# An attention and two MLPs on one core: the first eight heads' first queries as whole float32 products, the first MLP's operations at other places, and 40 unread products at the start

## The chip, the cores and the metric

The kernel runs on one core of a Trainium2 chip. The time is the device time of one execution in microseconds (us). Three executions of the kernel before took 917.24, 921.59 and 922.11 us; their median, 921.59 us, is what the changed kernel is compared with. Lower is better.

## The reference

Inputs are float32. Attention has 4 batches of 8 heads, 576 positions and a head size of 64; its output is the input of the first MLP, and that MLP's output the input of the second.

```python
cum = np.cumsum(np.maximum(s, 0.0), axis=-1)
scores = q @ k.T / 8 + np.minimum(-(cum[..., :, None] - cum[..., None, :]), 0.0)
attn = softmax(np.where(causal, -1e9, scores))       # over the keys
x = (attn @ v), transposed to 2304 tokens x 512
# first MLP: 512 -> 1024 -> 512
h = x @ w_in
solu = h * softmax(h)
x = (layernorm(solu) * g_ln) @ w_out
# second MLP: 512 -> 2048 -> 512
h = x @ w2_in
out = (h * np.clip(h + 3, 0, 6) / 6) @ w2_out
```

## The kernel before

ScalarE (ACT in the profile) writes the high part, and VectorE (DVE) or GpSimd (POOL) the low part. For queries and keys this is `split_qk` (ACT L1124, then POOL L610 and L613), for values `split_v` (POOL L627, L629), for the transposed probabilities `copy_probs` (ACT L1155) and `split_probs` (DVE L953), for the first MLP's weights `split_w_in` and `split_w_out`, and for its input `split_x` (DVE L1004 writes `xs_hi`, POOL L655 `xs_lo`).

**Units, items, slots.** A unit is a pair of heads with their first 256 queries (first kind) or the other 320 (second kind). A batch has four units of the first kind and then four of the second. A unit of the first kind has two items and one of the second five, 112 items in all. Each engine runs the same loop over slots n. In slot n TensorE transposes the probabilities of item n (`transpose_probs`, L736), multiplies them with the values of earlier units (`weighted_values`, L761) and computes the scores of item n+2 (L717, L720 and L722; L720 adds the causal mask). VectorE adds the decay bias and takes the row maximum of item n+1 (`row_max`, L944), and ScalarE takes the exponentials of item n+1 (`exp_row`, L1132). ScalarE and VectorE add up the two parts of the output (`copy_corr` L1163, `add_parts` L973), and a unit's output is scaled two slots after its last item (`scales_slot`). Each engine works strictly through its own list and waits on semaphores.

**The first MLP** is woven into the same loop: 18 steps t of 128 tokens, each cut in six pieces r = 0 to 5 on the slots that `STARTS` gives. Pieces 0 to 2 are `hidden` (L794, 24 products in a step). The row maximum (`max1`) comes in piece 3, the exponential (`exp1`, ACT L1182) and `solu` (DVE L1014 to L1022) in piece 4, and the squares (`square`, ACT L1188) in piece 5. The norm and the transposes (L807) follow in the next step, and pieces 3 to 5 hold the projection of an earlier pair of steps (`project`, L823). The second MLP follows as a loop of its own after the slots; all its products lie in L843 to L862.

A step's input can be split no earlier than the unit that completes its tokens is scaled:

```python
X_AT = {max(STARTS[t] - 3, whole_at(t)): t for t in range(NT)}
SPLIT_X_AT = {n + 1: t for n, t in X_AT.items()}
```

VectorE makes `xs_hi` in slot `X_AT`, and GpSimd makes `xs_lo` one slot later. `whole_at` is slot 10 for t = 0, slot 30 for t = 2, slot 58 for t = 6 and slot 114 for t = 15; `STARTS` of these four steps are 12, 31, 59 and 115. For the other steps the start lies four to eighteen slots behind `whole_at`.

**The start.** SyncE (SP) issues all loads. The bias of the first unit is spread over the partitions by two products (L869) after the cumulative sum (L923); all later ones are loaded from DRAM (`load_bias`).

Of the kernel before, what the change touches and what calls it, by code (L numbers as in the profile page):

```python
# [14 lines left out]
P = 128  # L15
# [63 lines left out]
A_WORDS = 4 * DH + 6 * ST + 6 * NQ * DH + 2 * BANK + SEQ + 3 * P + BANK + NQ * P + 2 * P_COLS  # L79
# [4 lines left out]
STARTS = [12, 21, 31, 37, 44, 51, 59, 65, 71, 77, 84, 90, 96, 102, 109, 115, 121, 127, 133]  # L84
# [10 lines left out]
W_IN_FROM, W_OUT_FROM, EARLY_FROM = 3, 24, 120  # L95

OWN = HEADS
# [18 lines left out]

def half_of(u):

    return u % 2 if FIRST_KIND[u] else 0

def units_of_half(u):

    return [m for m in range(u + 1) if half_of(m) == half_of(u)]

def load_of(u, e):
    return 2 * u + e
# [11 lines left out]
def buffer_of(load):  # L140

    return 3 + load if load < OWN else (load - OWN) % 3

def loads_of_buffer(load):

    return 1 if load < OWN else (load - OWN) // 3 + 1
# [10 lines left out]
for _u in range(UNITS):  # L158
    for _e in range(2):
        if load_of(_u, _e) < OWN:  # L160
            _n = max(-3, load_of(_u, _e) - 5)
        elif _u == PAIRS:
# [9 lines left out]
for _u in range(UNITS):  # L172
    for _e in range(2):
        VALUES_SLOT[_u, _e] = BASE[_u] + (1 + _e if not FIRST_KIND[_u] else _e)
        VALUES_AT.setdefault(VALUES_SLOT[_u, _e], []).append((_u, _e))
# [17 lines left out]
def build(nc, qk0, qk1, v_rows, s, w_in, w_out, g_ln, w2_in, w2_out, cum_dram, out):  # L193
    with ExitStack() as ctx:
# [27 lines left out]

# [17 lines left out]
        v_sp = [sb(a_region, f"v_sp{p}", [P, NQ, 2, DH], F32R) for p in range(2)]  # L241
        v_raw = [sb(a_region, f"v_raw{p}", [P, NQ, DH]) for p in range(2)]
        bias = [sb(a_region, f"bias{p}", [P, BANK]) for p in range(2)]
# [3 lines left out]
        p_hi = sb(a_region, "p_hi", [P, P_COLS], F32R)  # L247
        with ExitStack() as early:
            cum = sb(early, "cum", [NH, SEQ])
            s_pos = sb(early, "s_pos", [NH, SEQ])  # L250
        p_lo = sb(a_region, "p_lo", [P, P_COLS], F32R)
# [5 lines left out]
        with ExitStack() as own:  # L257
            for p in range(3, 3 + OWN):
                qk_buffer(own, p, QW[1] + KN[1])
# [10 lines left out]
        es = sb(first, "es", [P, F1])  # L270
        xs_hi = sb(first, "xs_hi", [P, NC, P], F32R)
# [95 lines left out]
        qk_loaded = [sem(f"qk_loaded{p}") for p in range(3 + OWN)]  # L367

        v_loaded = [[sem(f"v_loaded{p}{i}") for i in range(2)] for p in range(2)]
        bias_loaded = [[sem(f"bias_loaded{p}{i}") for i in range(2)] for p in range(2)]  # L370
        bias_tail_loaded = sem("bias_tail_loaded")
        w_in_loaded = [sem(f"w_in_loaded{p}") for p in range(W_IN_PARTS)]
        w_out_loaded = sem("w_out_loaded")
# [17 lines left out]
        pT_ready = sem("pT_ready")  # L391
        pT_hi_done = sem("pT_hi_done")
# [13 lines left out]
        bias_spread = sem("bias_spread")  # L406
        bias_copied = sem("bias_copied")
# [48 lines left out]
        def bias_loads(u):  # L456

            return len(units_of_half(u)) - (1 if half_of(u) == half_of(0) else 0)
# [7 lines left out]
        def _(sp):  # L466
            def load_qk(u, e):
                load = load_of(u, e)
                p, c = buffer_of(load), kind(u)
                if load >= OWN + 3:  # L470

                    u_, e_ = (load - 3) // 2, (load - 3) % 2
                    if FIRST_KIND[u_] or e_ == 1:
                        sp.wait_ge(scores_ready, BASE[u_] + (e_ if FIRST_KIND[u_] else 4) + 1)
                    else:
                        sp.wait_ge(tail_half_ready, sum(not k for k in FIRST_KIND[:u_ + 1]))
# [3 lines left out]
            def load_bias(u, e):  # L480
                before = user_before(u)
# [4 lines left out]
                sp.dma_start(bias[e][:, at:at + n], cum_dram[h:h + 1, 0:n].to_broadcast([P, n])).then_inc(bias_loaded[e][half_of(u)], 16)  # L486
# [9 lines left out]

            def load_v(u, e):
                before = user_before(u)
                if before >= 0:
# [15 lines left out]
            load_qk(0, 0)  # L515
            load_qk(0, 1)
            load_qk(1, 0)
            sp.wait_ge(cum_done, 1)
            sp.dma_start(cum_dram, cum[:, :]).then_inc(cum_stored, 16)
            load_qk(1, 1)  # L520
            sp.wait_ge(cum_stored, 16)
            for e in range(2):
                load_bias(1, e)
            load_qk(2, 0)
            for e in range(2):
                load_v(0, e)
            load_qk(2, 1)
            load_qk(3, 0)
            for e in range(2):
# [784 lines left out]
```

## Time and profile before

| | |
|---|---|
| three executions | 917.24, 921.59, 922.11 us |
| median | 921.59 us |
| profiled execution | 918.19 us, of which span 916.4 us |
| TensorE (PE) busy | 845.5 us, 92% of the span |
| VectorE busy | 441.9 us, 48% |
| ScalarE busy | 412.8 us, 45% |
| GpSimd busy | 296.5 us, 32% |
| mean granted clock of TensorE | 0.976 |

The span runs from the first to the last instruction, and 1.8 us of the execution lie around it. The slots with the attention and the first MLP fill about the first 508 us, and the second MLP the rest.
### The profile page before, as it was taken

The numbers are of one execution on the slowest core, as the hardware profiler recorded it, in microseconds if no ns is written. First come the engines' busy times: TensorE is split into PE (matmuls) and PEld (weight loads), VectorE is DVE, ScalarE is ACT, GpSimd is POOL, SyncE is SP. The second block draws the span as 40 slices with busy tenths as digits, with TensorE's granted clock in tenths as the row PEclk, the third lists the DMA queues.
The fourth block names the chain that finished last, engine by engine and source line by source line (L and its number), as shares of the span: only waits on it lengthen the run. The fifth ranks groups of instructions, "written<-read, shape, count | busy, mean of one in ns | idle before, by whom it ended". The sixth has DMA issues, their size and how long they took to land.

```text
span 916.4 us, 13790 instructions
## 1 busy us (share of the span) xinstructions
PE 845.5 (92%) x4916; PEld 750.7 (82%) x4916; DVE 441.9 (48%) x1061; ACT 412.8 (45%) x911; POOL 296.5 (32%) x391
## 2 busy tenths in 40 slices
PE   7778779989899998999898999999999999999997
PEld 5566668888688887888787999989898999999996
DVE  3747767776676767667455232232322232332222
ACT  6745766657566566555223243232322232322222
POOL 7764466455644465453165253000000000000000
PEclk9789879999999999999999999999999999999999
DMA  7536434334434344331402040000000000000000
GB/s 232 176 111 208 119 97 141 96 99 125 124 95 115 91 115 123 108 113 40 137 2 92 1 138 1 35 1 1 35 0 1 35 1 1 35 1 1 35 1 34
DMA packets 39426, 66.84 MB, mean 73 GB/s; under 512 B 4480, under 2 KB 16512, under 8 KB 39360
## 3 DMA queue, kind: packets, MB, share of 16 engines
q1 hardware_dynamic: 39360, 65.97, 23.7%
q8 instruction: 40, 0.66, 0.3%
q14 instruction: 26, 0.21, 0.1%
HBM read 61.16 MB, written 4.79 MB: 72 GB/s over the span
## 4 chain that ended last, share of the span: by engine, by line
PE 69%; DVE 10%; ACT 9%; issue 5%; POOL 4%; DMA 2%; SPq 0%; DVEq 0%; ACTq 0%; POOLq 0%
PE psum L794 9%; PE psum L843 7%; PE psum L845 7%; PE psum L861 7%; PE psum L844 7%; PE psum L862 7%; PE psum L860 7%; PE psum L761 4%; PE psum L823 3%; PE psum L736 3%; ACT prob L1132 3%; ACT p_hi L1155 2%; DVE es L1018 2%; PE psum L807 2%; PE psum L722 2%
## 5 line engine op out<-in xcount | busy, mean ns | idle before, releaser
L1086 DVE SCALAR_TENSOR_TENSOR act<-act,psum 128x384 f32<-128x384 f32 x96 | 53.2, 554 | 286.8 <-ACT act L1240 286.8
L1240 ACT ACTIVATE act<-psum,three 128x384 f32<-128x384 f32 x96 | 55.9, 582 | 285.7 <-PE psum L845 285.7
L843 PE MATMUL psum<-x_hi,w_hi 128*128 128x384 f32 x384 | 129.5, 337 | 0.9 <-DVE x_lo L1044 0.9
L845 PE MATMUL psum<-x_hi,w_lo 128*128 128x384 f32 x384 | 129.5, 337 | 0.0
L844 PE MATMUL psum<-x_lo,w_hi 128*128 128x384 f32 x384 | 129.0, 336 | 0.0
L862 PE MATMUL psum<-w_hi,g_lo 128*128 128x512 f32 x288 | 113.9, 395 | 0.0
L861 PE MATMUL psum<-w_lo,g_hi 128*128 128x512 f32 x288 | 113.7, 395 | 0.0
L860 PE MATMUL psum<-w_hi,g_hi 128*128 128x512 f32 x288 | 112.0, 389 | 0.0
L953 DVE TENSOR_TENSOR p_lo<-psum,p_hi 128x512 fp32r<-128x512 f32 (+2 forms) x128 | 71.9, 572 | 79.5 <-ACT p_hi L1155 79.0
L1155 ACT ACTIVATE p_hi<-psum 128x512 fp32r<-128x512 f32 (+2 forms) x128 | 62.3, 500 | 96.0 <-PE psum L736 63.1
L610 POOL TENSOR_TENSOR qk_hi<-qk_raw,qk_hi 64x256 fp32r<-64x256 f32 (+1 forms) x64 | 57.0, 891 | 125.3 <-ACT qk_hi L1124 124.1
L823 PE MATMUL psum<-lnT_hi,w_out_hi 128*128 128x256 f32 x288 | 83.2, 289 | 9.9 <-DVE xT L1040 9.7
L1132 ACT ACTIVATE prob<-prob,nmax 128x128 f32<-128x128 f32 (+4 forms) x144 | 83.2, 580 | 12.2 <-DVE nmax L944 12.0
L736 PE MATMUL psum<-ident,prob 128*128 128x128 f32 x400 | 67.9, 290 | 20.7 <-ACT prob L1132 17.6
L823 PE MATMUL psum<-lnT_lo,w_out_hi 128*128 128x256 f32 x288 | 82.2, 285 | 0.0
L823 PE MATMUL psum<-lnT_hi,w_out_lo 128*128 128x256 f32 x288 | 82.2, 285 | 0.0
L736 PEld LDWEIGHTS psum<-ident,prob 128*128 128x128 f32 x400 | 49.3, 147 | 33.2 <-ACT prob L1132 28.4
L843 PEld LDWEIGHTS psum<-x_hi,w_hi 128*128 128x128 f32 x384 | 72.1, 188 | 5.3 <-DVE x_lo L1044 1.1
L844 PEld LDWEIGHTS psum<-x_lo,w_hi 128*128 128x128 f32 x384 | 72.1, 188 | 4.0
L722 PE MATMUL psum<-qk_lo,qk_hi 128*128 128x128 f32 (+2 forms) x192 | 73.8, 388 | 0.0
L794 PE MATMUL psum<-w_in_hi,xs_hi 128*128 128x512 f32 x144 | 60.9, 423 | 12.7 <-POOL xs_lo L655 12.7
L613 POOL TENSOR_TENSOR qk_lo<-qk_raw,qk_hi 128x256 fp32r<-128x256 f32 (+1 forms) x64 | 70.9, 1108 | 5.0
(95 smaller groups left out, 1881.6 us busy)
## 6 DMA issues: line engine op xcount, KB each, us to landing
qk_raw<-qk SPq DMA_DIRECT2D x32, 480.0 KB, 3.5
qk_raw<-qk SPq DMA_DIRECT2D x32, 256.0 KB, 2.7
bias<-cum_dram SPq DMA_DIRECT2D x32, 256.0 KB, 3.9
v_raw<-v_rows SPq DMA_DIRECT2D x32, 160.0 KB, 3.1
bias_tail<-cum_dram SPq DMA_DIRECT2D x32, 144.0 KB, 3.8
out<-out_sb SPq DMA_DIRECT2D x6, 768.0 KB, 3.5
w_raw<-w_in SPq DMA_DIRECT2D x16, 256.0 KB, 3.2
w_raw<-w_out SPq DMA_DIRECT2D x16, 256.0 KB, 4.1
```

The source lines that it names most:

```text
L722: last = pe.matmul(ps, q, qk_lo[p][:, keys], start=False, stop=(part != 0))
L736: last = pe.transpose(dst, prob[:, src:src + P], ident[:, :])
L794: last = pe.matmul(bank(h_bank(t) + half), x, w, start=(n % 12 == 0), stop=(n % 12 == 11))
L823: last = pe.matmul(bank(L_BANK, PJW), w, x, start=(n == 0), stop=(n == 23))
L843: pe.matmul(ps, w2_hi[f][:, cols], xh, start=(c_ == 0), stop=False)
L844: pe.matmul(ps, w2_hi[f][:, cols], xl, start=False, stop=False)
L845: last = pe.matmul(ps, w2_lo[f][:, cols], xh, start=False, stop=(c_ == NC - 1))
L860: pe.matmul(bank(4 + k), gh, w2_hi[f][:, NC * P:], start=(f == 0), stop=False)
L861: pe.matmul(bank(4 + k), gh, w2_lo[f][:, NC * P:], start=False, stop=False)
L862: last = pe.matmul(bank(4 + k), gl, w2_hi[f][:, NC * P:], start=False, stop=(f == NF2 - 1))
L1132: sc.activation(p, p, ACT.Exp, scale=-1.0, bias=nmax[:, u % 2, col:col + 1], accum_out=rsum[:, u % 2, col:col + 1]).then_inc(exp_done, 1)
L1155: sc.activation(hi, ps, ACT.Copy).then_inc(pT_hi_done, 1)
```

## The change

Three things are changed together.

**Plain units.** The first four units (`PLAIN = 4`; batch 0, all eight heads, first 256 queries) are no longer split. Their queries and keys are loaded as float32 with the two heads of a pair on top of each other (`qk_plain`, 128 partitions) in place of each head twice. TensorE multiplies whole float32 operands with 64 rows, and the bias comes in as a further product of `cum_parts` (high and low part of the cumulative sum) with a column of `heads`. The probabilities are copied once, by VectorE (`copy_plain`), and multiplied as float32 with the loaded values (`v_pair`). The output is copied once, by ScalarE (`copy_sums`), and `add_parts` falls away. The two products L869 and their copies go, the full cumulative sum is made after the first `copy_plain` (`sum_all`), and the loads come in another order.

**First MLP.** `STARTS` changes. In the slots `exp1` and `square` come behind the copy of the probabilities and the exponentials; `max1` and `solu` come right behind `row_max`, and `solu` in piece 5 in place of 4. `square` writes to SBUF (`squares`), and `hidden` waits for `solu` in place of `square`. `w_out` is loaded in eight parts of 256 KB in place of one of 2048 KB and split in slots 27 to 34 (24 to 31 before); `w_in` is split in slots 6 to 13 (3 to 10 before).

**Head of the program.** TensorE begins with 40 products of 128 columns whose result nobody reads.

```diff
-STARTS = [12, 21, 31, 37, 44, 51, 59, 65, 71, 77, 84, 90, 96, 102, 109, 115, 121, 127, 133]
+STARTS = [13, 25, 33, 39, 45, 54, 60, 66, 72, 78, 84, 90, 96, 103, 110, 116, 122, 129, 135]
-W_IN_FROM, W_OUT_FROM, EARLY_FROM = 3, 24, 120
+W_IN_LOAD = 2
+W_IN_FROM = 6
+W_OUT_LOAD = 15
+W_OUT_FROM = 27
+PLAIN = 4
...
+                    if u < PLAIN:
+                        rows = slice(0, P) if e is None else slice(e * DH, (e + 1) * DH)
+                        q = qk_plain[u][rows, q_at:q_at + P]
+                        for lo_, hi_ in [(0, w)] if w <= BANK else [(0, w // 2), (w // 2, w)]:
+                            pe.matmul(psum[:, at + lo_:at + hi_], q, qk_plain[u][rows, QW[c] + lo_:QW[c] + hi_],
+                                      start=True, stop=False)
+                            if n <= 1:
+                                pe.wait_ge(cum_parts_done, n + 1)
+                            h = head_of(u, e)
+                            last = pe.matmul(psum[:, at + lo_:at + hi_], heads[rows, h:h + 1].broadcast_to([DH, P]),
+                                             cum_parts[rows, lo_:hi_], start=False, stop=hi_ <= diag0)
...
+                    if u < PLAIN:
+                        p, v_at = plain_values(u)
+                        last = pe.matmul(psum[:, o_at + q:o_at + width], v_pair[p][:, v_at + j, :, :].rearrange("p a d -> p (a d)"),
+                                         p_plain[:, src:src + width - q], start=(j == 0), stop=(j == blocks - 1))
...
-                    wait(pe, sq_done, t - 1 if t >= NT - 2 else t)
+                    wait(pe, solu_done, t - 1 if t >= NT - 2 else t)
...
-            pe.wait_ge(cum_done, 1)
-            for e in range(2):
-                pe.matmul(bank(H_BANK + e, CUT), ident[0:NH, e:e + 1].broadcast_to([NH, P]), cum[:, 0:CUT],
-                          start=True, stop=True).then_inc(bias_spread, 1)
+            for _ in range(40):
+                pe.matmul(bank(H_BANK + 1, P), ident_bf[:, :], mask_bf[:, :], start=True, stop=True)
...
+                if r == 3:
+                    max1(t)
+                if r == 5:
+                    solu(t)
...
-                if 0 <= n < ITEMS:
+                if 0 <= n < PLAIN_ITEMS:
+                    copy_plain(n)
+                    if n == 0:
+                        sum_all()
+                elif 0 <= n < ITEMS:
                     split_probs(n)
...
-                if r == 3:
-                    max1(t)
-                if r == 4:
-                    solu(t)
```

TensorE's list at its start, before (L869 spreads the bias; `qk_hi3` and `qk_lo3` are parts of one head's queries and keys):

```order
L869 MATMUL psum<-cum,ident 128x256 x2
L717 MATMUL psum<-qk_hi3 128x128
L720 MATMUL psum<-mask_bf,ident_bf 128x128
L722 MATMUL psum<-qk_lo3,qk_hi3 128x128
L717 MATMUL psum<-qk_hi3 128x256
L720 MATMUL psum<-mask_bf,ident_bf 128x128
L722 MATMUL psum<-qk_lo3,qk_hi3 128x256
```

The same place in the changed kernel (L974 are the unread products, L796 the float32 ones, L801 the bias):

```order
L974 MATMUL psum<-mask_bf,ident_bf 128x128 x40
L796 MATMUL psum<-qk_plain0 128x128
L801 MATMUL psum<-cum_parts,heads 128x128
L805 MATMUL psum<-mask_bf,ident_bf 128x128
L796 MATMUL psum<-qk_plain0 128x256
L801 MATMUL psum<-cum_parts,heads 128x256
L805 MATMUL psum<-mask_bf,ident_bf 128x128
```

For each tile one float32 product and one bias product stand where two float32r products stood.

ScalarE's list around the first step's exponential, before (L1182 is `exp1`, L1155 and L1132 the attention's copy and exponential):

```order
L1132 ACTIVATE prob,rsum<-prob,nmax 128x384
L1182 ACTIVATE es,esum1<-psum,nmax1 128x1024
L1155 ACTIVATE p_hi<-psum 128x3x128
L1132 ACTIVATE prob,rsum<-prob,nmax 128x512
L1163 ACTIVATE xT<-psum 64x320
L1124 ACTIVATE qk_hi0<-qk_raw0 128x960
L1188 ACTIVATE psum,sq_sum<-es,neg_mu 128x1024
L1155 ACTIVATE p_hi<-psum 128x4x128
```

The same operations in the changed kernel, at the third step (L1328 is `exp1`, L1296 and L1273 the attention's):

```order
L1296 ACTIVATE p_hi<-psum 128x384
L1273 ACTIVATE prob,rsum<-prob,nmax 128x128
L1273 ACTIVATE prob,rsum<-prob,nmax 128x256
L1328 ACTIVATE es,esum1<-psum,nmax1 128x1024
L1265 ACTIVATE qk_hi1<-qk_raw1 128x512
L1322 ACTIVATE w_out_hi<-w_out_raw,g_sb 128x512
L1296 ACTIVATE p_hi<-psum 128x384
```

The exponential of the MLP stood ahead of the slot's attention work and now stands behind it.

VectorE's list at the first step's `solu`, before (L1014 to L1022 are `solu`, L953 is the low part of the probabilities, L944 the row maximum):

```order
L944 ISA prob,nmax<-psum,bias0 128x512
L944 ISA nmax 128x1
L953 TENSOR_TENSOR p_lo<-psum,p_hi 128x3x128
L973 TENSOR_TENSOR xT<-psum,xT 64x320
L959 TENSOR_SCALAR den<-rsum 128x5
L963 RECIPROCAL rden<-den 128x5
L1014 TENSOR_SCALAR den1<-esum1 128x1
L1016 RECIPROCAL rden1<-den1 128x1
L1018 SCALAR_TENSOR_TENSOR es,solu_sum<-psum,rden1,es 128x1024
L1022 TENSOR_SCALAR neg_mu<-solu_sum 128x1
```

The same place in the changed kernel (L1150 to L1158 are `solu`, L1089 the low part, L1062 the row maximum):

```order
L1062 ISA prob,nmax<-psum,bias00 128x512
L1062 ISA nmax 128x1
L1150 TENSOR_SCALAR den1<-esum1 128x1
L1152 RECIPROCAL rden1<-den1 128x1
L1154 SCALAR_TENSOR_TENSOR es,solu_sum<-psum,rden1,es 128x1024
L1158 TENSOR_SCALAR neg_mu<-solu_sum 128x1
L1089 TENSOR_TENSOR p_lo<-psum,p_hi 128x3x128
L1109 TENSOR_TENSOR xT<-psum,xT 64x320
```

`solu` stood behind the low part of the probabilities and now stands ahead of it.

## Rows read from the trace of the kernel before

**Rows 1.** The page, busy time of each engine.
```profile
PE 845.5 (92%) x4916; PEld 750.7 (82%) x4916; DVE 441.9 (48%) x1061; ACT 412.8 (45%) x911; POOL 296.5 (32%) x391
```

**Rows 2.** Stretches: bounds, length, busy time by engine, PEclk, DMA share, GB/s.
```profile
11.00:22.10 11.10, 9.69 (x44) 8.15 (x43) 5.32 (x21) 9.34 (x28) 8.98 (x18) 1.00 0.90 292
...
49.40:56.20 6.80, 5.02 (x13) 3.67 (x14) 0.00 (x0) 0.00 (x0) 2.95 (x3) 0.50 0.03 8
...
104.00:110.90 6.90, 4.62 (x21) 4.21 (x20) 5.35 (x18) 4.69 (x14) 4.05 (x6) 0.51 0.43 125
...
117.70:127.90 10.20, 6.27 (x21) 5.16 (x22) 7.31 (x19) 5.42 (x15) 8.32 (x14) 0.50 0.20 53
...
233.70:237.10 3.40, 3.40 (x11) 2.60 (x10) 0.18 (x1) 0.00 (x0) 2.19 (x4) 0.50 0.00 0
...
452.20:455.60 3.40, 3.40 (x12) 2.71 (x10) 0.00 (x0) 0.00 (x0) 0.00 (x0) 0.50 1.00 350
...
508.00:910.00 402.00, 402.00 (x2044) 364.79 (x2043) 111.33 (x215) 116.15 (x227) 23.97 (x10) 1.00 0.05 18
```

**Rows 3.** Waits, whole span: total us, times, longest.
```profile
PE psum L736 <- ACT prob L1132: 17.6, 23, 2.3
PE psum L794 <- POOL xs_lo L655: 12.7, 4, 3.8
...
ACT psum L1188 <- DVE neg_mu L1022: 37.0, 17, 3.1
...
ACT es L1182 <- DVE nmax L1009: 26.5, 15, 2.8
```

**Rows 4.** Timeline of TensorE: start, length, instruction; transposes of slots 0, 2, 3, 8.
```profile
9.90 0.90 PE L736 MATMUL psum<-ident,prob 128*128 128x128 f32 x3 [0.30 <-ACT prob L1132]
...
15.34 0.90 PE L736 MATMUL psum<-ident,prob 128*128 128x128 f32 x3 [0.22 <-ACT prob L1132]
...
17.70 0.90 PE L736 MATMUL psum<-ident,prob 128*128 128x128 f32 x3 [0.22 <-ACT prob L1132]
...
34.19 0.84 PE L736 MATMUL psum<-ident,prob 128*128 128x128 f32 x3
```

**Rows 5.** Timeline of ScalarE in slot 2.
```profile
16.28 0.49 ACT L1155 ACTIVATE p_hi<-psum 128x384 fp32r<-128x384 f32 x1 [0.47 <-PE psum L736]
...
17.55 0.62 ACT L1124 ACTIVATE qk_hi<-qk_raw 128x512 fp32r<-128x512 f32 x1
```

**Rows 6.** Timeline of TensorE: float32 products, scores of head 0, values.
```profile
4.80 2.04 PE L869 MATMUL psum<-cum,ident 32*128 32x256 f32 x4 [4.80 <-DVE cum L923]
6.77 0.47 PE L717 MATMUL psum<-qk_hi 128*128 128x128 f32 x1
...
8.16 0.31 PE L717 MATMUL psum<-qk_hi 128*128 128x128 f32 x1
...
18.25 0.56 PE L761 MATMUL psum<-p_hi,v_sp 128*128 128x256 f32 x1
...
19.14 0.52 PE L761 MATMUL psum<-p_hi,v_sp 128*128 128x256 f32 x1
```

**Rows 7.** Timeline of TensorE: the four waits for `xs_lo`.
```profile
51.18 0.80 PE L794 MATMUL psum<-w_in_hi,xs_hi 128*128 128x512 f32 x1 [3.77 <-POOL xs_lo L655]
...
124.15 0.79 PE L794 MATMUL psum<-w_in_hi,xs_hi 128*128 128x512 f32 x1 [2.95 <-POOL xs_lo L655]
...
233.38 0.51 PE L794 MATMUL psum<-w_in_hi,xs_hi 128*128 128x512 f32 x1 [3.56 <-POOL xs_lo L655]
...
451.64 0.50 PE L794 MATMUL psum<-w_in_hi,xs_hi 128*128 128x512 f32 x1 [2.42 <-POOL xs_lo L655]
```

**Rows 8.** Timeline of GpSimd ahead of the first of these waits' end.
```profile
48.51 1.40 POOL L613 TENSOR_TENSOR qk_lo<-qk_raw,qk_hi 128x576 fp32r<-128x576 f32 x1
49.87 1.26 POOL L655 TENSOR_TENSOR xs_lo<-xT,xs_hi 128x512 fp32r<-128x512 f32 x1
```

**Rows 9.** Chain that ended last: one `hidden` piece of eight products.
```profile
455.78 1.86 PE psum L794 x8
```

**Rows 10.** Timeline of VectorE: the long instruction of `solu`.
```profile
446.59 1.28 DVE L1018 SCALAR_TENSOR_TENSOR es<-psum,rden,es 128x1024 f32<-128x1024 f32 x1
```

More of the change, by code:

```diff
@@ L140, in buffer_of, with los, seconds, plain_values @@
 def buffer_of(load):
-    return 3 + load if load < OWN else (load - OWN) % 3
+    return load % 3
 def loads_of_buffer(load):
-    return 1 if load < OWN else (load - OWN) // 3 + 1
+    return load // 3 + 1
+def los(n):
+    return LOS_BEFORE[n] - LOS_BEFORE[PLAIN_ITEMS]
+def seconds(u):
+    return sum(not k for k in FIRST_KIND[PLAIN:u + 1])
+def plain_values(u):
+    if FIRST_KIND[u]:
+        return u // 2 % 2, u % 2 * 2
+    return u % 2, 0
 SUMS_AT = {}
@@ L157 @@
 SPLIT_AT = {}
-for _u in range(UNITS):
+for _u in range(PLAIN, UNITS):
     for _e in range(2):
-        if load_of(_u, _e) < OWN:
-            _n = max(-3, load_of(_u, _e) - 5)
-        elif _u == PAIRS:
+        if _u == PLAIN:
             _n = BASE[_u] - 5 + _e
@@ L190, with build @@
 SPLIT_X_AT = {n + 1: t for n, t in X_AT.items()}
-def build(nc, qk0, qk1, v_rows, s, w_in, w_out, g_ln, w2_in, w2_out, cum_dram, out):
+def build(nc, qk0, qk1, plain0, plain1, v_rows, v_pairs, s, w_in, w_out, g_ln, w2_in, w2_out, cum_dram, out):
     with ExitStack() as ctx:
@@ L257, in build @@
         with ExitStack() as own:
-            for p in range(3, 3 + OWN):
-                qk_buffer(own, p, QW[1] + KN[1])
+            qk_plain = [sb(own, f"qk_plain{u}", [P, QW[kind(u)] + KN[kind(u)]]) for u in range(PLAIN)]
         w_out_hi = sb(first, "w_out_hi", [P, NF1, DM], F32R)
@@ L456, in bias_loads @@
         def bias_loads(u):
-            return len(units_of_half(u)) - (1 if half_of(u) == half_of(0) else 0)
+            return sum(bias_place(m) == bias_place(u) for m in range(PLAIN, u + 1))
         def tokens(u):
@@ L475, in load_qk @@
                     else:
-                        sp.wait_ge(tail_half_ready, sum(not k for k in FIRST_KIND[:u_ + 1]))
+                        sp.wait_ge(tail_half_ready, seconds(u_))
                 w = QW[c] + KN[c]
@@ L549, in _ @@
                             load_bias_tail(u)
-                for u in range(2, UNITS):
+                for u in range(PLAIN, UNITS):
                     for e in range(2):
@@ L1211, in _ @@
                 t, r = STEP_AT.get(n, (None, None))
[L1212 to L1216 removed]
+                if PLAIN_ITEMS <= n < ITEMS:
                     copy_probs(n)
@@ L1221, in _ @@
                 for u, e in SUMS_AT.get(n, ()):
-                    copy_corr(u, e)
+                    if u < PLAIN:
+                        copy_sums(u, e)
+                    else:
+                        copy_corr(u, e)
+                if r == 4:
+                    exp1(t)
+                if r == 5:
+                    square(t)
                 if r in (1, 2) and t >= 1:
                     copy_ln(t - 1, r - 1)
+                for u, e in SPLIT_AT.get(n, ()):
+                    split_qk(u, e)
                 if W_OUT_FROM <= n < W_OUT_FROM + NF1:
@@ L1289, with pairs @@
     values = np.concatenate([v, np.zeros((NH, NQ * P - SEQ, DH), np.float32)], axis=1)
+    values = values.reshape(NH, NQ, P, DH).transpose(0, 2, 1, 3)
+    def pairs(x):
+        return x[:HEADS].reshape(PAIRS, 2 * DH, x.shape[2])
+    first = np.concatenate([qT[:, :, :CUT], kT[:, :, :CUT]], axis=2)
+    second = np.concatenate([qT[:, :, CUT:cut], tails, kT], axis=2)
     def twice(x):
@@ L1295 @@
     arrays = {
-        "qk0": twice(np.concatenate([qT[:, :, :CUT], kT[:, :, :CUT]], axis=2)),
-        "qk1": twice(np.concatenate([qT[:, :, CUT:cut], tails, kT], axis=2)),
-        "v_rows": values.reshape(NH, NQ, P, DH).transpose(0, 2, 1, 3),
+        "qk0": twice(first),
+        "qk1": twice(second),
+        "plain0": pairs(first),
+        "plain1": pairs(second),
+        "v_rows": values,
+        "v_pairs": values[:HEADS].reshape(PAIRS, 2, P, NQ, DH).transpose(0, 2, 3, 1, 4),
         "s": s.reshape(NH, SEQ),
```

259 lines of the change are left out of this document (166 added, 93 removed).

## The prediction

> **What bounds the kernel now.** The page comes first: TensorE is busy 92% of the span and no other engine reaches half [rows 1]. A table of stretches then shows that this share is made of two parts. From 508 to 910 us TensorE is busy 402.00 of 402 us at full clock [rows 2]; that is the second MLP, which the change leaves as it is. What can be won lies in the slots, the first 508 us. There TensorE loses time in two ways, and both have rows. It waits: 17.6 us for exponentials of the attention and 12.7 us for `xs_lo` of the first MLP [rows 3]. And it runs at half clock, 1.2 GHz: six named stretches [rows 2]. In 11.0 to 22.1 us products run at the half-clock spacing (a slot's scores and transposes repeat every 2.36 us, 15.34 to 17.70 [rows 4]); the table's 1.00 there only means that no change had been recorded. The other five stretches of half clock come behind idle time: 49.4 to 56.2 behind a wait of 3.77 us, 233.7 and 452.2 inside or just behind waits of 3.56 and 2.42 us [rows 2, 7].
>
> The timeline of the first slots shows a closed loop: ScalarE copies the transposed probabilities 0.47 us after the transposes are done, then takes two exponentials, 1.27 us from 16.28 to 17.55 [rows 5], and TensorE's next transposes wait for these. Nine slots' starts, slot 0 at 9.90 and slot 8 at 34.19, are 24.3 us apart [rows 4].
>
> **Term 1, slots 0 to 8.** The copy of the probabilities leaves ScalarE, so its exponentials no longer wait for the transposes, and the loop is cut. ScalarE also loses eight splits of queries and keys of 0.62 us [rows 5], GpSimd all its work for these heads, and SyncE loads half the bytes of queries and keys in a stretch whose transfers fill 0.90 of the DMA engines [rows 2]. What binds then is TensorE itself. Two float32 products of 256 columns started at 4.80, and the next product could start at 6.77 [rows 6], so one costs up to 0.98 us at half clock; I take 0.95, and 0.48 for 128 columns. A head's scores then cost 0.48 + 0.95 for the products, about 0.55 for two bias products and 0.18 for two masks (both from the 1.39 us that six products took, 6.77 to 8.16 [rows 6]), 2.2 us in place of 1.39. A head's values cost 0.95 + 0.48 = 1.4 us in place of 0.89 (18.25 to 19.14 [rows 6]). With transposes (0.55) and scales a slot holds 4.2 us of TensorE at half clock and 2.1 us at full clock, 1.3 and 0.65 us more than before. These are the two bounds: 8 x 2.1 + 1.5 us of starting latency = 18.3 us, a gain of 6.0; or 8 x 4.2 + 1.5 = 35.1 us, a loss of 10.8. Which of them comes is the clock's affair. The 40 products need no data, can start when the constants are there, and end about when the first scores can start; behind them TensorE's list is dense for the first time in this program. Before, it was busy 9.69 of 11.1 us in short products and rose to full clock only at 22.1. I take the full clock, -6.
>
> The Trainium skill (FP8 and Floating Point Precision, TensorE Precision Notes) says that true float32 takes four passes through the array. By it 256 columns would be 4 x 256 / 1.2 GHz = 0.85 us, and the eight slots at half clock an estimated 2 us cheaper than by the row. The row agrees within what stands between the two products.
>
> **Term 2, slots 8 to 13.** Before, slot 8 began at 34.19 and the first `hidden` piece at 51.18, behind a wait of 3.77 us [rows 4, 7]; GpSimd was late, with queries' low part and `xs_lo` back to back until 51.1 [rows 8]. It enters this stretch with no backlog now, and the step starts in slot 13, three behind `whole_at` 10, not two. The wait goes, 3.8 us, and its eight products run at full clock, another 1.8 us (they took 1.86 us elsewhere [rows 9]). The splits of `w_in` that now lie here add to ScalarE what they took three slots earlier before; I take 0.6 back. -5.
>
> **Term 3, the other waits for `xs_lo`.** They stand at t = 2, 6 and 15, 2.95 + 3.56 + 2.42 = 8.9 us [rows 7]. These are exactly the steps that started one slot behind `whole_at`, the slot in which GpSimd only makes `xs_lo`. The new starts lie 3, 2 and 2 slots behind. Between nothing (the wait moves along, if all that TensorE has in the added slot is done early) and all 8.9, I take -7, since a slot holds a piece of TensorE work of 1.9 us [rows 9] besides the attention.
>
> **Term 4, half clock behind them.** In the stretches from 104.0, 117.7, 233.7 and 452.2 TensorE is busy 4.62 + 6.27 + 3.40 + 3.40 = 17.7 us at half clock [rows 2]; all at full clock would give 8.8. With fewer and shorter waits I take -5; the lower bound is nothing.
>
> **Term 5, ScalarE's list.** `square` and `exp1` hold ScalarE back 37.0 and 26.5 us in waits [rows 3], with the attention's copy and exponentials behind them. Put behind these they cost the attention nothing. But only 17.6 us of TensorE's time hang on exponentials, a part of them in the first slots. -3, between 0 and -10. The load of `w_out` in parts shortens no wait that I find on the chain: 0. Unread products end before the first scores: 0.
>
> **Term 6, work moved later.** Steps 0 to 2 ended in slot 36 and now end in slot 38. Two pieces of 1.9 us leave a stretch where TensorE waits in any case and are done where it is full: +4.
>
> **Sum.** -6 - 5 - 7 - 5 - 3 + 4 = -22. The profiled execution took 918.2 us, and gives 896. It lies 3.4 us below the median, from which the sum gives 900. I say 898.
>
> **Rivals.**
> *The first slots stay at half clock.* For it: 9.69 us busy of 11.1 did not raise the clock before. Against: float32 products stream four times the columns. Term 1 turns from -6 to +11: 915. Chance 0.12.
> *The waits move along and ScalarE binds.* Slots 8 to 36 are full of exponentials, splits and copies, so TensorE, with less to do there, waits for them at half clock; terms 3 to 5 give -5 rather than -15: 908. Chance 0.12.
> *The other side, slower.* `solu` (1.28 us [rows 10] and three short instructions, some 1.8 us) now stands ahead of the low part of the probabilities, for which the next transposes wait; so are late the exponentials' consumers behind them. Fifteen steps share slots with attention: up to 27 us. Where all of it reaches TensorE the sum is +5, 925. It decides from about 1.5 us a step. Against: ScalarE's copy, which the low part needs too, covers about 0.9 us, and TensorE has a 1.9 us projection piece in that slot. Chance 0.08.
> *More comes back.* All waits of terms 3 to 5 and all half clock: -37, 883. Chance 0.08.
>
> **Numbers.** The likeliest case has 0.60, and its own range is 889 to 907. The range 882 to 916 holds it and the first two rivals and leaves out the slower one. Half a per cent, 4.6 us, is what a measurement here can tell from no change. Faster than 917 are the likeliest case, most of the first two rivals and the last: 0.87. Within 0.5% the edge of the first rivals: 0.06. Slower 0.07.
>
> **What would show it.** Slot 8's transposes near 28 us, not near 43; products at full spacing from about 8 us on. ScalarE's waits before `square` and `exp1` nearly gone. No wait for `xs_lo` of over 1 us, and no fall of the clock at the starts of steps 2, 6 and 15. The last slot ending some 20 us before 508, and then 402 us as before. Wrong would make me: half clock until 20 us; VectorE late with the low part in the slots of piece 5, seen as a wait of the transposes for it; or new waits of TensorE for exponentials in slots 13 to 36.

## The result, and the profile after

The changed kernel takes 882.36 us (median of 4 runs: 881.93, 882.01, 882.71 and 890.40), the kernel before 921.84 us beside it. The ratio is 0.9604, with a 95% interval of 0.9541 to 0.9666: 39 us faster, where the prediction said 898 and a range of 882 to 916. The profiled execution took 882.01 us, with a span of 880.2; its counterpart before took 918.19, so the two traces differ by 36 us.

The page of the changed kernel, busy time of each engine; beside it stands [rows 1]:

```profile
PE 839.7 (95%) x4968; PEld 748.3 (85%) x4968; DVE 435.9 (50%) x1059; ACT 405.9 (46%) x893; POOL 282.0 (32%) x361
```

TensorE is busy 6 us less in a span that is 36 us shorter: what went is idle time, and busy time at half clock. Its stretches (bounds, length, busy time by engine, PEclk, DMA share, GB/s); beside them [rows 2]:

```profile
7.00:28.20 21.20, 20.91 (x123) 15.57 (x123) 12.73 (x53) 12.99 (x42) 5.96 (x7) 1.00 0.65 220
40.70:47.50 6.80, 6.07 (x20) 5.47 (x21) 2.50 (x8) 3.73 (x9) 4.99 (x5) 0.50 0.35 109
95.30:102.10 6.80, 6.32 (x30) 5.50 (x29) 6.25 (x20) 5.48 (x16) 4.46 (x8) 0.50 0.32 83
105.50:115.70 10.20, 7.10 (x27) 6.08 (x28) 6.87 (x21) 7.71 (x20) 7.83 (x12) 0.50 0.35 113
457.10:460.50 3.40, 3.37 (x11) 3.37 (x12) 1.06 (x2) 0.00 (x0) 0.00 (x0) 0.50 0.13 49
470.00:872.00 402.00, 402.00 (x2048) 364.99 (x2048) 111.46 (x216) 116.23 (x227) 24.02 (x10) 1.00 0.05 18
```

Full clock comes at 6.5 us instead of 22.1. The stretches of half clock at 233.7 and 452.2 are gone. One at the first step (40.7) and two in slots 29 to 33 (95.3 and 105.5) remain. The one at the start of the second MLP (457.1) is new; before, the clock stood at full there. The window of 402 us in the second MLP is again busy 402.00 of 402. The whole of it is longer than that window. Its first product came at 494.89 before, not at 508, and comes at 457.13 now:

```profile
494.89 0.45 PE L843 MATMUL psum<-x_hi,w_hi 128*128 128x384 f32 x1 [0.93 <-DVE x_lo L1044]
457.13 0.69 PE L949 MATMUL psum<-x_hi,w_hi 128*128 128x384 f32 x1 [2.60 <-DVE x_lo L1180]
```

So the slots are 37.8 us shorter, and what follows them is 1.6 us longer. Waits over the whole span (total us, times, longest), to be set beside [rows 3]:

```profile
ACT squares L1334 <- DVE neg_mu L1158: 14.6, 7, 4.3
PE psum L834 <- ACT prob L1273: 8.9, 13, 1.7
ACT es L1328 <- DVE nmax L1145: 7.9, 3, 2.9
PE psum L834 <- DVE p_lo L1089: 7.5, 6, 3.4
PE psum L929 <- DVE xT L1176: 5.3, 11, 0.6
PE psum L949 <- DVE x_lo L1180: 2.6, 1, 2.6
PE psum L900 <- POOL xs_lo L723: 0.8, 1, 0.8
```

The wait for `xs_lo` falls from 12.7 to 0.8 us, that for exponentials from 17.6 to 8.9. The low part of the probabilities is a wait that grew, from 2.5 us to 7.5. Three more rows of the kernel before, for the readings below:

```profile
PE psum L717 <- DVE nmax L944: 5.5, 5, 2.3
...
PE psum L773 <- DVE xT L973: 4.1, 6, 1.3
PE psum L736 <- DVE p_lo L953: 2.5, 3, 1.1
```

The first is TensorE's scores waiting for `row_max`, the second its products behind `add_parts`.

The timeline of TensorE at slots 0 and 8 (as [rows 4]) and at the starts of steps 0, 2, 6 and 15 (as [rows 7]):

```profile
10.12 0.55 PE L834 MATMUL psum<-ident,prob 128*128 128x128 f32 x3
...
28.25 0.49 PE L834 MATMUL psum<-ident,prob 128*128 128x128 f32 x3
...
44.41 0.77 PE L900 MATMUL psum<-w_in_hi,xs_hi 128*128 128x512 f32 x1
...
113.56 0.73 PE L900 MATMUL psum<-w_in_hi,xs_hi 128*128 128x512 f32 x1
...
212.39 0.48 PE L900 MATMUL psum<-w_in_hi,xs_hi 128*128 128x512 f32 x1
...
413.48 0.40 PE L900 MATMUL psum<-w_in_hi,xs_hi 128*128 128x512 f32 x1
```

No bracket stands behind the four products: none waits. Set against the trace before, slot 8 is 5.9 us early, step 0 6.8, step 2 10.6, step 6 21.0, step 15 38.2. So 17 us of the gain lie between steps 6 and 15 (212 to 413 us), where no head is plain and where the sum had only the wait of step 15 (2.42 us), the half clock behind the start of step 6 (1.7) and a part of term 5's 3 us.

### The profile page after: what moved, and what is told of

The parts are those of the page before. It is cut to its first block, busy times and chain, and to the rows that moved or that the text cites. A ratio compares the mean times of both kernels' runs of the same rounds, so it can differ in the third digit from the quotient of the medians.

```text
span 880.2 us, 13819 instructions
## 1 busy us (share of the span) xinstructions
PE 839.7 (95%) x4968; PEld 748.3 (85%) x4968; DVE 435.9 (50%) x1059; ACT 405.9 (46%) x893; POOL 282.0 (32%) x361
## 4 chain that ended last, share of the span: by engine, by line
PE 81%; ACT 7%; DVE 5%; issue 3%; POOL 3%; DMA 1%; ACTq 0%; DVEq 0%; POOLq 0%
PE psum L929 9%; PE psum L900 9%; PE psum L949 8%; PE psum L951 8%; PE psum L950 8%; PE psum L967 8%; PE psum L968 8%; PE psum L966 7%; PE psum L867 5%; PE psum L834 4%; PE psum L818 2%; PE psum L813 2%; ACT prob L1273 2%; PE psum L913 2%; ACT p_hi L1296 1%
## 5 line engine op out<-in xcount | busy, mean ns | idle before, releaser
L1296 ACT ACTIVATE p_hi<-psum 128x384 fp32r<-128x384 f32 (+1 forms) x120 | 58.7, 503 | 100.9 <-PE psum L834 66.5
L1273 ACT ACTIVATE prob<-prob,nmax 128x128 f32<-128x128 f32 (+4 forms) x144 | 83.4, 580 | 22.8 <-DVE nmax L1062 22.2
L1089 DVE TENSOR_TENSOR p_lo<-psum,p_hi 128x384 fp32r<-128x384 f32 (+1 forms) x120 | 67.1, 571 | 53.7 <-ACT p_hi L1296 53.7
L679 POOL TENSOR_TENSOR qk_hi<-qk_raw,qk_hi 64x384 fp32r<-64x384 f32 (+1 forms) x56 | 50.5, 901 | 103.3 <-ACT qk_hi L1265 101.7
L834 PE MATMUL psum<-ident,prob 128*128 128x128 f32 x400 | 64.8, 280 | 16.5 <-ACT prob L1273 8.9
L951 PEld LDWEIGHTS psum<-x_hi,w_lo 128*128 128x128 f32 x384 | 72.4, 189 | 0.0
L834 PEld LDWEIGHTS psum<-ident,prob 128*128 128x128 f32 x400 | 47.5, 143 | 26.7 <-ACT prob L1273 17.5
L682 POOL TENSOR_TENSOR qk_lo<-qk_raw,qk_hi 128x576 fp32r<-128x576 f32 (+1 forms) x56 | 67.7, 1208 | 4.4
L818 PE MATMUL psum<-qk_lo,qk_hi 128*128 128x288 f32 (+4 forms) x176 | 65.1, 375 | 0.0
```

Source lines behind the costliest of these rows:

```text
L682: pool.tensor_tensor(qk_lo[p][:, k_cols], qk_raw[p][:, k_cols], qk_hi[p][:, k_cols].bitcast(F32), ALU.subtract).then_inc(k_lo_done, 1)
L818: last = pe.matmul(ps, q, qk_lo[p][:, keys], start=False, stop=(part != 0))
L834: last = pe.transpose(dst, prob[:, src:src + P], ident[:, :])
L951: last = pe.matmul(ps, w2_lo[f][:, cols], xh, start=False, stop=(c_ == NC - 1))
L1273: sc.activation(p, p, ACT.Exp, scale=-1.0, bias=nmax[:, u % 2, col:col + 1], accum_out=rsum[:, u % 2, col:col + 1]).then_inc(exp_done, 1)
```

## The experiments

Each run was timed in up to five rounds beside the kernel before (medians of 919.3 to 921.8). The table has them all; the ratio is to the kernel before. The changed kernel has 0.9604 [0.9541, 0.9666]; its interval is wide because of its one run at 890.40, so differences of 5 us to it rest on the medians and on its other three runs.

| kernel | us | ratio, 95% interval |
|---|---|---|
| before + lists | 906.9 | 0.9845 [0.9823, 0.9868] |
| before + starts | 908.8 | 0.9864 [0.9844, 0.9884] |
| before + lists + starts | 888.0 | 0.9654 [0.9630, 0.9678] |
| the same + unread products | 890.1 | 0.9670 [0.9647, 0.9692] |
| changed, no unread products | 887.7 | 0.9656 [0.9630, 0.9681] |
| changed, old starts | 906.8 | 0.9865 [0.9835, 0.9895] |
| changed, old lists | 901.1 | 0.9806 [0.9766, 0.9846] |
| changed, ScalarE's list old | 910.2 | 0.9880 [0.9845, 0.9915] |
| changed, VectorE's list old | 902.8 | 0.9785 [0.9762, 0.9808] |
| changed, `solu` behind the low part | 891.7 | 0.9717 [0.9679, 0.9755] |
| changed, `split_x2` first | 886.0 | 0.9623 [0.9602, 0.9645] |
| the same, 24 more unread | 878.6 | 0.9540 [0.9520, 0.9560] |

**The new lists and starts alone.** The kernel before with the new lists and starts (its transposes' wait is written for the bank that each uses, since the first step now begins at an odd slot). It lacks the plain heads and the unread products, and also the smaller parts of the change: `square` into SBUF, `w_out` in eight parts, the later `w_in`. None of these smaller parts was timed alone.

```
-STARTS = [12, 21, 31, 37, ...
+STARTS = [13, 25, 33, 39, ...
 ScalarE:  -exp1, square ahead of copy_probs     +behind copy_corr
 VectorE:  -max1 (r 3), solu (r 4) behind invert +max1 (r 3), solu (r 5) ahead of split_probs
```

> The kernel before with two parts of the change alone: the new list of starts of the first MLP's steps, and the new places of `exp1`, `square`, `max1` and `solu` in the lists of ScalarE and VectorE. The first eight heads stay split, `square` still writes to PSUM, no unread products. By the terms of the prediction (3, 4, 5 and 6: -7 - 5 - 3 + 4) it gains 11 us on the kernel before, so 911, and the first heads hold the other 28 of the 39 us measured. The rival says that the order of the lists was priced too low: the two changed traces differ by 12 us more in slots 60 to 112 than the terms allow, where no plain head is; then this kernel gains 22 to 27 us, 895 to 900, and the first heads hold only the 11 us of terms 1 and 2.

It took 888.0, so it gains 31 us, three times the -11 of the terms and more than the rival's 22 to 27. Its waits:

```profile
PE psum L736 <- ACT prob L1132: 11.4, 19, 1.1
PE psum L736 <- DVE p_lo L953: 7.3, 6, 3.1
...
PE psum L823 <- DVE xT L1040: 3.1, 6, 0.6
...
PE psum L794 <- ACT psum L1188: 1.2, 1, 1.2
...
PE psum L794 <- POOL xs_lo L655: 0.8, 1, 0.8
```

They are nearly those of the changed kernel. The wait of `hidden` for `square` (L1188) is one that the changed kernel lacks, since its `hidden` waits for `solu`. Its first slots are those of before (slot 8 at 34.3), and the 6 us that it lacks to the changed kernel come from there: slot 12 stands 7.8 us behind the changed kernel's, slot 108 4.9, and the wait of 1.2 for `square` comes at 419.8.

**Each of the two alone.**

> The kernel before with the new places of `exp1`, `square`, `max1` and `solu` alone; old starts, split heads, `square` into PSUM, no unread products. Lists and new starts together gave 31 us. If each holds its own part, as the prediction's sum has it, this kernel and the one with the new starts alone add up to 31: by term 5 this one gives 3 us, 916; by the cost of taking the lists back out of the changed kernel (19 us, 6 of them in the first slots' clock) it gives 13: 906. The rival: they only pay together, since with steps one slot behind `whole_at` the waits for `xs_lo` stay whatever the lists; then it gives under 8 us, 912 to 919.

> The kernel before with the new list of starts alone (its transposes' wait is written for the bank that each uses, as in the changed kernel, since the first step now begins at an odd slot). By terms 3, 4 and 6: -7 - 5 + 4, 8 us, 911. By what was missing after the lists (31 less 13): 18 us, 901. No wait for `xs_lo` of over 1 us at steps 1, 2, 6 and 15 in either. The rival that they only pay together: 912 to 919.

The lists alone gain 14 us, the starts alone 12, and together 31: each has most of its worth alone, and 5 us come only with both. The waits of the kernel with the lists alone:

```profile
PE psum L794 <- POOL xs_lo L655: 12.6, 5, 3.5
PE psum L736 <- ACT prob L1132: 9.3, 14, 1.5
PE psum L736 <- DVE p_lo L953: 7.9, 7, 2.7
...
PE psum L823 <- DVE xT L1040: 3.3, 6, 0.6
```

The wait for `xs_lo` is untouched (12.7 before). Those for exponentials fall from 17.6 [rows 3] by 8.3 us. And waits fall that the prediction left out: that of the scores for `row_max` from 5.5 to 0.8, that behind `add_parts` (4.1) to nothing, and that of projections for `copy_x2` by 6.4 us, from this row of the kernel before:

```profile
PE psum L823 <- DVE xT L1040: 9.7, 12, 1.5
```

Against them the wait for the low part rises from 2.5 to 7.9.

The waits of the kernel with the starts alone:

```profile
PE psum L736 <- ACT prob L1132: 23.0, 25, 2.5
PE psum L823 <- DVE xT L1040: 9.2, 13, 1.4
...
PE psum L794 <- POOL xs_lo L655: 2.3, 2, 1.2
```

Here 10 us of waits for `xs_lo` went and 5 us of waits for exponentials came. This is the rival "the waits move along and ScalarE binds", and it is real as long as ScalarE has the old list. One of the two waits for `xs_lo` that stay is step 15's, 1.23 us at 441.57, where the expectation allowed no more than 1.

**The same two, taken out of the changed kernel.**

> The changed kernel with the old lists: `exp1` and `square` stand ahead of the attention's copy and exponentials on ScalarE, `max1` and `solu` behind the attention's work on VectorE, `solu` in piece 4 again. Plain heads, new starts and the unread products stay. Term 5 of the prediction prices the lists at 3 us: 885 to 886. The rival (lists priced too low) says 10 to 15 us: 892 to 898, with the waits of `square` back near 37 us and those of `exp1` near 26 us, and the loss spread over all steps rather than at their starts.

> The changed kernel with the old list of starts, but 13 for the first step (old: 12). Terms 3, 4 and 6 say that waits for `xs_lo` of up to 3.5 us come back at steps 2 and 6 and one of 2.4 at step 15, with half clock behind them, less the 4 us of work moved later: 8 us slower than the changed kernel, 890. The rival: the waits came from a slow GpSimd and ScalarE in the split heads and the old lists, which this kernel does not have; then xs_lo is in time even one slot behind, and the time is 880 to 884.

The old lists cost 19 us (901.1); the waits of `square` are 36.6 us again, those of `exp1` 26.2. The profiled execution took 905.1, 23 us more than the changed kernel's; in it the clock fell in the first slots (below), which is worth about 5 of the 23. The rest is spread as the rival had it: slots 60 to 108 take 192.8 us in place of 178.4. These slots in the changed kernel:

```profile
211.90:390.30 178.40, 175.50 (x1239) 157.20 (x1238) 132.87 (x346) 118.15 (x273) 101.41 (x139) 1.00 0.39 113
```

The same slots of the kernel with the old lists:

```profile
223.20:416.00 192.80, 178.95 (x1238) 158.69 (x1239) 132.99 (x349) 118.41 (x273) 99.28 (x138) 0.99 0.34 105
```

And TensorE's waits in it:

```profile
PE psum L929 <- DVE xT L1176: 9.1, 8, 1.8
PE psum L879 <- DVE xT L1109: 2.9, 3, 1.3
PE psum L834 <- ACT prob L1273: 1.0, 3, 0.4
```

TensorE's busy time differs by 3.5 us, its idle time by 11. And only 1.0 us of its idle time is a wait for exponentials. 12 of 13.9 us are waits for VectorE, for `copy_x2` and for the sums. VectorE itself stands in `split_probs` for `p_hi`, which ScalarE makes behind `exp1`. Its wait in these slots, with the old lists and then in the changed kernel:

```profile
DVE p_lo L1089 <- ACT p_hi L1296: 36.5, 36, 2.3
DVE p_lo L1089 <- ACT p_hi L1296: 23.3, 26, 2.5
```

That this wait is what makes `copy_x2` late is read from the order of VectorE's list, in which `copy_x2` of piece 4 comes right behind the low part.

The old starts cost 24 us (906.8), but 5.7 of it is a wait of the experiment's own: step 2 begins two slots earlier, and its first projection waits for `w_out_lo`, whose place was not moved. Waits for `xs_lo` are back at 9.4 us, and 23.9 us in a row run at half clock from 95.9. In its profiled execution, too, the clock fell in the first slots. Both theories priced it too low.

**One list at a time.** In the changed kernel one engine's list is put back, the other stays.

> The changed kernel with ScalarE's list alone put back: `exp1` and `square` ahead of the attention's copy and exponentials; VectorE's list stays new. If the loss of the old lists came through ScalarE (a wait at the head of its list delays the copy of the probabilities, so VectorE's low part, so the copies of x2 behind it, so the projections), most of the 18 us come back here: `max1` is early now, so `exp1` hardly waits, but `square` waits some 2 us a step for `solu`, which the same slot makes: 892 to 898. The rival: VectorE's own order is what matters, and this kernel takes 882 to 886.

> The changed kernel with VectorE's list alone put back: `max1` behind the attention's work in piece 3, `solu` behind it in piece 4; ScalarE's list stays new. The piece-5 slots then have no `solu` ahead of the low part. If that place cost something (the prediction's slower rival), this kernel is faster than the changed one by up to the waits for `p_lo`, 7.5 us: 875 to 882. If `solu` in piece 4 waits for an `exp1` that now stands at the end of ScalarE's list, VectorE stands some 2 us a step before the next slot's maximum, and it takes 887 to 898.

Both are worse than expected. With ScalarE's list alone put back the kernel takes 910.2, more than with both (901.1); with VectorE's alone 902.8, which is not to be told from both by the intervals, and where the slowest expectation ended at 898. Waits with ScalarE's list put back:

```profile
ACT squares L1334 <- DVE neg_mu L1158: 56.8, 18, 4.3
ACT es L1328 <- DVE nmax L1145: 7.9, 3, 2.9
...
PE psum L834 <- ACT prob L1273: 23.0, 21, 4.0
PE psum L929 <- DVE xT L1176: 5.3, 11, 0.6
```

`square` at the head of ScalarE's slot waits in every step for a `solu` of the same slot, 3.2 us on average (37.0 before in 17 waits), and the attention's copy and exponentials wait with it. The waits for `copy_x2`, though, are the changed kernel's 5.3 us: `max1` is early here, so `exp1` at the head of its slot hardly waits (7.9). It takes both halves of the old lists, `max1` late and `exp1` early, to delay `copy_x2`. With VectorE's list put back another wait grows, that of ScalarE's exponentials for the row maximum, 22.2 us in the changed kernel:

```profile
ACT prob L1273 <- DVE nmax L1062: 48.5, 45, 5.9
```

The two lists are one edit: `solu` may come early only where `square` comes late.

**Where `solu` stands on VectorE.**

```
                 if r == 3:
                     max1(t)
-                if r == 5:
-                    solu(t)
 ...
                 elif 0 <= n < ITEMS:
                     split_probs(n)
+                if r == 5:
+                    solu(t)
```

> The changed kernel with one line moved on VectorE: `solu` still in piece 5, but directly behind the low part of the probabilities instead of ahead of it. The prediction's slower rival said that `solu` ahead of the low part costs TensorE time. In the changed kernel's trace it does so at one place by 3.4 us (slot 31, piece 5 of step 1: the low part ends at 106.77 though its high part is there since 103.4), and the clock falls behind it; all waits for the low part come to 7.5 us. If these go and nothing takes their place: 876 to 879. The rival: `square` now waits longer for `solu` at the end of ScalarE's list, and the next slot's copy of the probabilities with it, as in the two kernels with one list put back; then 882 or above, up to 890.

It took 891.7, 9 us slower; four of six runs lie within 891.4 to 891.7. The other two took 900.6 and 900.7, and the trace is one of these, with 20.5 us of half clock in the first slots. In the changed kernel `solu` does hold up the low part in slot 31. TensorE's and VectorE's timeline there:

```profile
104.82 1.28 DVE L1154 SCALAR_TENSOR_TENSOR es<-psum,rden,es 128x1024 f32<-128x1024 f32 x1
...
106.22 0.55 DVE L1089 TENSOR_TENSOR p_lo<-psum,p_hi 128x384 fp32r<-128x384 f32 x1
...
106.92 0.88 PE L834 MATMUL psum<-ident,prob 128*128 128x128 f32 x3 [3.35 <-DVE p_lo L1089]
```

With `solu` behind, this slot takes 4.4 us instead of 6.0 (100.9 to 106.9). But the next takes 6.4 instead of 4.4, with a wait of 2.13 us for exponentials at its end: `square` comes later on ScalarE, then two splits, then `p_hi`. The wait moved and did not go. Over the whole kernel `square` waits 33.6 us (18 times) instead of 14.6 (7 times).

**The first slots and the clock.**

> The changed kernel without the 40 unread products at the head of TensorE's program, nothing else. If they are what brings the full clock to the first slots, the granted clock stays at 1.2 GHz beyond 6.5 us as long as the first slots' products do not raise it, and slot 8's transposes come later than 28.3: up to 43 us if it lasts through eight slots. If the plain products alone raise it, it rises 3 to 4 us after the first of them at about 7 us, and the loss is at most 1.5 us: 882 to 884, not to be told from the changed kernel by its time, but by slot 8's transposes at 29 to 30.

> The kernel before with the new lists and new starts (888.0) and the 40 unread products ahead of TensorE's first wait; the eight heads stay split. This asks whether the first heads' gain is the clock's alone. In this kernel's parent eight slots took 24.4 us, 34.3 at slot 8, and slots 4 to 8 were no faster than 0 to 4 though most of them ran at full clock. If ScalarE's loop sets the pace whatever the clock, slot 8 comes 2.3 us later, since the 40 products end at about 7.1 and the products that spread the bias start at 4.8 now: 36 to 37, and the time is 889 to 891. If the clock sets the pace, slot 8 comes at 31 to 32, and the time is 884 to 886, and the plain heads have little part in the gain.

The changed kernel without the unread products takes 887.7, with slot 8 at 37.0. Its first scores run at half clock though they start at 4.13, and the clock rises only at 31.0: from a product of 256 columns to the next instruction it is 0.34 us at 7.62 in the changed kernel, and 0.65 here. The split heads with unread products take 890.1, with slot 8 at 34.0, as without them (34.3). But the products didn't hold the clock there:

```profile
10.00:33.90 23.90, 22.02 (x94) 18.70 (x95) 14.89 (x52) 19.39 (x57) 20.34 (x34) 0.50 0.83 258
```

The same heads in the kernel without these products had full clock in a part of slots 4 to 8:

```profile
23.00:29.80 6.80, 4.20 (x30) 3.18 (x29) 5.44 (x16) 5.53 (x17) 6.40 (x9) 1.00 0.80 255
```

These four slots took 12.8 us in both. So where split heads had full clock they were no faster, and ScalarE's loop paced them there; eight split slots at full clock were seen in no trace. On top of the new lists and starts (0.9654) the rest of the change without unread products gives nothing (0.9656), nor do unread products alone (0.9670). All together gives 5.6 us in the medians (0.9604), which the intervals don't separate from nothing; three of four runs of the changed kernel lie at 881.9 to 882.7, and all of the three others at 886.8 or above.

**The head's clock is not settled by the 40 products.** Seven profiled executions ran kernels with the same first slots (the expectation below says six, and four falls; the count is seven and five). In two, the changed kernel's among them, the clock held from 7 us to about 40. In five it fell again between 10.3 and 11.6. The stretches of the kernel with `split_x2` first:

```profile
7.00:10.00 3.00, 3.00 (x19) 2.17 (x17) 0.64 (x4) 0.68 (x3) 0.00 (x0) 1.00 0.63 238
10.40:24.10 13.70, 13.70 (x47) 9.83 (x47) 6.12 (x24) 4.38 (x18) 0.40 (x1) 0.50 0.72 208
```

and of the same kernel with 24 more unread products:

```profile
7.00:10.00 3.00, 3.00 (x27) 2.33 (x25) 0.64 (x4) 0.99 (x4) 0.00 (x0) 1.00 0.68 257
10.40:24.10 13.70, 13.70 (x92) 10.55 (x90) 8.88 (x37) 8.79 (x29) 3.82 (x5) 1.00 0.69 193
```

The first of these kernels answers another question as well: the wait of 2.6 us for `x_lo` at the start of the second MLP.

```
+                if t == NT - 1 and r in (1, 2, 4, 5):
+                    split_x2(0, (1, 2, 4, 5).index(r))
                 if r == 4:
                     exp1(t)
                 if r == 5:
                     square(t)
```

(the same two lines ahead of `max1` on VectorE, and gone from their old places)

> The changed kernel with the split of the first transposed tokens for the second MLP (`split_x2`, four parts, in the last step alone) ahead of `exp1` and `square` on ScalarE and ahead of `max1` and `solu` on VectorE, instead of behind them. In the changed kernel its last part stands behind a wait of 3.20 us of `square` for `solu`; TensorE waits 2.60 us for it at 457.13 and then runs at half clock for 3.4 us. If that is the whole of it: the wait goes and the clock stays, 2.6 + 1.7 = 4.3 us, 878. The rival: the waits of the projection for the copies of x2 in the same step take its place, or the clock falls a little later: 881 to 883.

The wait and the half clock behind it are gone: from step 17's first product to the second MLP's first it takes 13.2 us instead of 16.0, and no fall of the clock stands there. But the median is 886.0, where 878 was expected. The first slots lost 6.2 us to the clock in the profiled execution, and the runs scatter, 882.3 to 887.3; the profiled one is the fastest of them. The last kernel adds, in TensorE's list:

```
                         scores(n + 2)
+                    if n < 0:
+                        for _ in range(12):
+                            pe.matmul(bank(H_BANK + 1, P), ident_bf[:, :], mask_bf[:, :], start=True, stop=True)
```

> The kernel with `split_x2` first, and 24 more unread products in TensorE's list: 12 behind the scores of slot 0 and 12 behind those of slot 1, 0.055 us each at full clock, 1.3 us in all. In six profiled executions of kernels with the same first slots the clock, up since about 7 us, fell again between 10.3 and 11.6 in four and held in two (the changed kernel's among them); where it fell slot 8 began at 34.4 or later in place of 28.3, and the end came some 5 us later. If the fall follows from too little work in the first scores, the added products hold the clock: slot 8 at 29.6 and 878 to 880 in nearly all runs. If it does not depend on them, the runs scatter as those of the kernel with `split_x2` first alone did, 882 to 887, plus up to 1.3: 883 to 889, and slot 8 stands at 29.6 or at 35.7 by the run.

All five runs lie between 877.6 and 879.8. In the profiled one slot 8 stands at 29.1, the clock holds until 40.0, and the 0.8 us that the products cost there have shrunk to 0.1 by slot 32. It beats the changed kernel by 4 us and the kernel before by 43. That the added work is what holds the clock follows from that one trace and from the narrow spread, beside a kernel that differs in nothing else and has no run below 882.3; which property of the products counts was not tried.

## Why the prediction was right, and where its terms were off

The direction, the mechanisms and the bound (TensorE's waits and half clock in the slots) were right. The sum of -22 was 14 us short of the profiled difference of 36. The rival "more comes back" gave 883 at a chance of 0.08, and that is what was measured, at the lower edge of the range. But the number was met in part by luck: that rival has all half clock gone, and some 24 us of it stayed in the slots (40.7, 95.3 and 105.5), while waits that no term names came on top.

**Terms 1 and 2, -6 and -5, measured -5.6 together (the smaller parts of the change included).** Slot 8 came at 28.25 as said, and step 0's wait went. But the starts alone, with the heads as before, take that wait too, so term 2 was counted to the wrong edit. Inside term 1 two errors cancelled: a head's scores take 1.54 us at full clock (6.98 to 8.52), not 1.1, and a slot 2.3, not 2.1, but the 1.5 us of starting latency did not come. At half clock a slot took 3.9 us (five from 9.44 to 28.80 without the unread products), not 4.2. "Unread products end before the first scores: 0" was wrong too: without them the first scores start at 4.13, with them at 6.98; they pay for that through the clock. The choice of full clock was luck in part: it holds in some executions and falls in others.

The Trainium skill (TensorE: Matmul & The Clock Gate, What's actually happening) says that the clock's rise is run-variable, since it depends on where the first products fall. The traces agree: in seven executions of the same first slots the first unread product started at 2.96 and the rise came between 6.5 and 8.2. The same section of the Trainium skill ties the slow state to idleness; here the clock fell at 10.4 with TensorE busy 3.00 of 3.00 us ahead of it, so busy time in the trace is not enough, and the measurement decides.

**Terms 3 and 4, -12, and term 6, +4.** The starts alone measured -12 against -8. The waits of steps 0, 2 and 6 went whole and half of step 15's (1.23 of 2.42 us stayed; in the changed kernel it is gone), the half clock at steps 6 and 15 too. Term 6 can't be told from the clock: slots 32 to 36 take 2.7 us more than before, but 8.8 us of them now run at half clock, which before ended where slot 32 began. The half clock at the start of step 2 stayed, and there the prediction was wrong: 105.5 to 115.7, from inside the wait of 3.35 us for the low part on, the one place where the slower rival's mechanism showed.

**Term 5, -3, measured -14 alone and -19 on top of the starts.** This is the step that failed. Its 16 us, with 4 from the starts and 5 less from the heads, are the missing 14 to within a microsecond. It said: "only 17.6 us of TensorE's time hang on exponentials". That read one wait of TensorE as all that ScalarE's waits can reach. But `p_hi` also feeds VectorE, and behind `split_probs` stand `copy_x2` and the sums. These cost TensorE 9.7 us for `copy_x2` alone, in a row of the kernel before that the prediction didn't bring. The lists alone took 8.3 us from the one wait, 6.4 from that one and 8.8 from two more that name VectorE (`row_max` 4.7, the sums 4.1), and gave 5.4 back in waits for the low part.

**The rivals.** First slots at half clock: real in five of seven profiled executions, but in four of them the clock was back at 24 us and slot 8 came at 34.4 to 34.6, where before had 34.2, and not near 43. That is worth about 5 us at the end, not 17. In the fifth it was back at 32.1, and slot 8 came at 38.0. Waits move along to ScalarE: true of the starts alone (+5.4 us of waits), prevented by the lists. The slower one: `solu` ahead of the low part costs one wait of 3.35 us and saves 9 us over the kernel.

## What to carry to other kernels

An instruction that waits at the head of an engine's list delays all behind it, and their consumers on other engines: price it by every wait that hangs on that list, through VectorE too, and not by the one that names the engine. Two lists that hand work to each other are moved together: here ScalarE's old list beside VectorE's new one cost 9 us more than both old, and the other way round it gained nothing on both old. Where a kernel's first slots are short products, look at several executions before the clock is credited with anything; here a microsecond of unread products brought five runs within 2.2 us of each other.

## What the hardware showed that was not expected

The granted clock fell at 10.3 to 11.6 us in five of seven profiled executions of the same first slots, in the one shown without a gap in TensorE's work, and stayed down 13.7 us (20.5 in one of them). In the kernel with `split_x2` first it cost 6.2 us at slot 8 and 4.7 at slot 60. From a float32 product of 256 columns with 64 rows to the next instruction's start it is 0.34 us at full clock and 0.65 at half, where the prediction had 0.48 and 0.95. That isn't its whole cost: a head's scores took 1.54 us at full clock against 1.1, so the bias and mask products behind it, or its own end, take more than the prediction gave them, and the trace doesn't say which.
